# The first chain reordered on every engine, with unread TensorE products in its waits, GpSimd's share of two base inverses recut, and half blocks transposed in turns

## The reference

```python
def _attn_ref(q, k, v, beta):                 # 4 batches, 8 heads, 768 tokens, head dim 48
    k_n = k / (np.linalg.norm(k, axis=-1, keepdims=True) + 1e-06)
    state = np.zeros((B, H, D, D)); y = np.zeros_like(q)
    for t in range(S):
        kt, vt, bt = (k_n[:, :, t], v[:, :, t], beta[:, :, t, None])
        y[:, :, t] = np.einsum('bhd,bhde->bhe', q[:, :, t], state)
        v_old = np.einsum('bhde,bhd->bhe', state, kt)
        state = state + bt[:, :, :, None] * np.einsum('bhd,bhe->bhde', kt, vt - v_old)
    return y
def _moe_ref(x, w1, w2, w3, w_out):           # x 3072 x 384, inner 768
    h = np.maximum(np.maximum(x @ w1, x @ w2), x @ w3)
    return h @ w_out
def _moe2_ref(x, w_gate, w_noise, noise, w1, w2):   # 8 experts, inner 1024
    noisy = x @ w_gate + np.log1p(np.exp(x @ w_noise)) * noise
    # the two best experts of each token, softmax weights over the two,
    # out[token] += weight * (relu(x @ w1[e]) @ w2[e])
```

## Time and profile before

| what | value |
|---|---|
| median of 3 runs | 1051.75 us (1051.23 to 1052.74) |
| the profiled execution: its time | 1057.48 us |
| its span, first to last instruction | 1055.7 us |
| mean granted clock of TensorE | 0.971 of full |
| PE busy | 998.3 us (95%), 10317 matmuls |
| DVE busy | 731.3 us (69%) |
| ACT busy | 475.3 us (45%) |
| POOL busy | 202.0 us (19%) |

### The profile page before, as it was taken

One profiled execution on the slowest core, in us unless ns is written; L12 is line 12 of the kernel. 1 busy time (PEld: TensorE's weight loads), 2 busy tenths in 40 slices (PEclk: granted clock), 3 DMA queues, 4 the chain that ended last, 5 costly groups with the idle time before them and its releaser, 6 DMA issues.

```text
span 1055.7 us, 25602 instructions
## 1 busy us (share of the span) xinstructions
PE 998.3 (95%) x10317; PEld 928.0 (88%) x10317; DVE 731.3 (69%) x1690; ACT 475.3 (45%) x707; POOL 202.0 (19%) x226
## 2 busy tenths in 40 slices
PE   5779988999999999999999999999999999999995
PEld 5667777889889889889899999999999999999994
DVE  5956596487578588442559776777677776776774
ACT  3511424423523523422255464556465464655553
POOL 0086000020022021022306312112111112212111
PEclk8589999999999999999999999999999999999998
DMA  9160131151141042025555645225162525536121
GB/s 320 45 161 2 37 87 21 45 142 21 31 140 37 2 113 52 6 75 200 181 195 188 141 95 152 62 44 173 31 172 46 150 53 165 162 56 165 38 38 23
DMA packets 71459, 102.03 MB, mean 97 GB/s; under 512 B 28624, under 2 KB 59856, under 8 KB 70992
## 3 DMA queue, kind: packets, MB, share of 16 engines
q1 hardware_dynamic: 59296, 78.51, 24.7%
q0 software_dynamic: 10992, 20.70, 10.3%
q10 hardware_dynamic: 1088, 1.65, 0.5%
HBM read 140.53 MB, written 29.51 MB: 161 GB/s over the span
## 4 chain that ended last, share of the span: by engine, by line
PE 84%; DVE 5%; ACT 4%; issue 2%; SPq 2%; DMA 2%; POOLq 0%; DVEq 0%; ACTq 0%
PE ps L1615 40%; PE ps L1761 21%; PE ps L1656 7%; PE ps L1498 3%; PE ps L1592 2%; PE ps L1582 2%; PE ps L1572 2%; PE ps L1672 2%; PE ps L1481 2%; PE ps L1533 1%; PE ps L1543 1%; SPq L446 1%; DVE joint L1040 1%; DMA noise_s<-in_noise 1%; PE ps L1602 1%
## 5 line engine op out<-in xcount | busy, mean ns | idle before, releaser
L1615 PE MATMUL ps<-xr,wr_in 128*128 128x512 f32 x972 | 239.0, 400 | 2.2 <-DVE xr L1070 2.1
L1761 PE MATMUL ps<-w2r,hbT 128*128 128x384 f32 x1320 | 237.0, 337 | 0.0
L1761 PEld LDWEIGHTS ps<-w2r,hbT 128*128 128x128 f32 x1320 | 227.9, 188 | 1.4 <-DVE hbT L1290 1.4
L1615 PEld LDWEIGHTS ps<-xr,wr_in 128*128 128x128 f32 x972 | 180.7, 190 | 42.6 <-DVE xr L1070 2.4
L1615 PE MATMUL ps<-xbT,w1r 128*128 128x256 f32 x1728 | 211.0, 283 | 0.0
L1615 PEld LDWEIGHTS ps<-xbT,w1r 128*128 128x128 f32 x1728 | 210.1, 192 | 0.0
L661 POOL DMA_INDIRECT out_rows<-yb,idx x55 | 90.5, 1646 | 379.8 <-DVE yb L1302 290.9
L1116 DVE TENSOR_TENSOR w1r<-w1s,w1r 128x768 fp32r<-128x768 f32 x128 | 121.2, 957 | 20.0 <-ACT w1r L798 17.7
L814 ACT ACTIVATE hbT<-ps 128x512 fp32r<-128x512 f32 x96 | 57.3, 597 | 169.2 <-PE ps L1615 166.8
L798 ACT CAST w1r<-w1s 128x768 fp32r<-128x768 f32 x128 | 104.4, 827 | 25.5 <-DMA w1s<-in_we 25.5
L1116 DVE TENSOR_TENSOR w2r<-w2s,w2r 128x768 fp32r<-128x768 f32 x128 | 113.8, 951 | 1.5 <-ACT w2r L802 1.5
(11 more groups left out here) (211 smaller groups left out, 1053.3 us busy)
## 6 DMA issues: line engine op xcount, KB each, us to landing
w1s<-in_we SPq DMA_DIRECT2D x32, 1536.0 KB
w2s<-in_we SPq DMA_DIRECT2D x32, 1536.0 KB
xb<-rows SPq DMA_DIRECT2D x25, 402.0 KB
kv_s<-in_kv SPq DMA_DIRECT2D x24, 384.0 KB, 3.3
k_s<-in_k SPq DMA_DIRECT2D x12, 512.0 KB, 3.7
joint<-in_q SPq DMA_DIRECT2D x24, 256.0 KB
out_rows<-padrow SPq DMA_DIRECT2D x13, 384.0 KB, 4.3
w_in<-in_w_blocks SPq DMA_DIRECT2D x3, 1152.0 KB, 12.0
```

Of the source, the lines that this page charges most:

```text
L1615: mm = pe.matmul(dst, w, m, start=(n == 0), stop=(n == len(todo) - 1))
L1761: mm = pe.matmul(ps[:, 6 + h, 0:MD], hbT[:, a, f, h * P:h * P + P], w2r[par][:, b, f], start=(f == 0 and n == 0), stop=(f == FT2 - 1 and n ...
```

## The change

In the opening the lists of all engines are put in another order, and TensorE gets `keep_warm` products: matmuls of a matrix of ones with itself into PSUM banks that nobody reads then. VectorE takes one half of the corner's copy (`corner_half`), ScalarE both halves of the copies after `solve_u(0)` and `outputs(0)`. `fold` no longer waits for the noise, and its loads are issued ahead of the first weights. GpSimd does the first 16 steps of pair 1's base and the first 24 of pair 2's (`POOL_STEPS`), VectorE the rest. In tile 0 the pair's work starts one slot later (`START`), and k1, u1 and s1 stand one slot earlier after it. The first product of tile 0 takes its high parts before the low parts are there. In half blocks `block_rows` stands between the two groups of transposes, and the output product takes the high parts first. The diff, cut to its core:

```diff
+        POOL_STEPS = {1: 16, 2: 24}
+        def base_before(cp):
+            return sum(STEPS - base_ops(POOL_STEPS.get(n, 0)) for n in range(cp))
+        def pool_base_before(cp):
+            return sum(2 * POOL_STEPS.get(n, 0) for n in range(cp))
-        START = {0: 7, 1: 1}
+        START = {0: 8, 1: 1}
-            tight = {... "u0": 6, "s0": 7, "k1": 9, "u1": 10, "s1": 11}
+            tight = {... "u0": 6, "s0": 7, "k1": 8, "u1": 9, "s1": 10}
         def base_done(n, t, i):
-            low, first = place(n - 1, "low"), place(n - 2, "gram1") + (3 if n == 2 else 4)
-            early = Q - 1 if n == 2 else 28
+            low, first = place(n - 1, "low"), place(n - 2, "gram1") + 4
+            early = POOL_STEPS.get(n, 28)
+            if t == 0 and n == 1:
+                return early + (Q - 1 - early) * min(max(i - 1, 0), low - 2) // (low - 2)
# SyncE: w_oT and w_gn now ahead of w_in (w_gn's semaphore is s_wT)
+            sp.dma_start(w_oT[:], w_out_t.rearrange("(k p) f -> p k f", p=P)).then_inc(s_wT, 16)
+            sp.dma_start(w_gn[:], w_gate_noise).then_inc(s_wT, 16)
             for f in range(0, FT, 2):
                 sp.dma_start(w_in[:, f:f + 2], w_blocks[:, f:f + 2]).then_inc(s_w, 16)
-            sp.dma_start(w_oT[:], ...).then_inc(s_wT, 16)
-            sp.dma_start(w_gn[:], w_gate_noise).then_inc(s_noise, 16)
# GpSimd: ones set first; base in parts
+            nc.gpsimd.memset(ones[:], 1.0).then_inc(s_padrow, 1)
-            def second_pair_base():
-                for k in range(Q - 1):
+            def pool_base(cp):
+                for k in range(POOL_STEPS[cp]):
-                if t == -1:
-                    second_pair_base()
+                if t + 2 in POOL_STEPS:
+                    pool_base(t + 2)
# ScalarE
-                for h_ in range(1 if c < 2 else 2):      # u_out, y_out
+                for h_ in range(1 if c == 1 else 2):
             solve_diagonals(0)
+            corner(0)                                    # one half of two
+            off_diagonals_of(3)
             off_diagonals_of(2)
-            off_diagonals_of(3)
             roots(1)
-            corner(0)
# VectorE
+            def corner_half():
+                dve.wait_ge(p_corner, 1)
+                dve.wait_ge(s_solve, 1)
+                rows = slice(L, L + Q)
+                nc.vector.tensor_scalar(by_bank_pair(solve[rows, :, Q:L]), ps[rows, E_BANKS:E_BANKS + 2, :]..., -1.0, None, ALU.mult)
             columns_of(0)
             norm_columns(0)
             scaled_v(0)
+            rows_of(1)
+            corner_half()
             pT_out(0)
-            rows_of(1)
+            norms(1)
             weights_low(0)
-            norms(1)
-            u_half(0)
             state_out(0)
-            y_half(0)
+            weights_low(1)
             scaled_v(1)
             r_out(1)
             pT_out(1)
             u_half(1)
             norm_columns(1)
+            weights_low(2)
             state_out(1)
-            weights_low(1)
             y_half(1)
+            weights_low(3)
             x_low(0)
-                    if t == 0 and n == 0 and f + 2 < FT:
-                        weights_low(f + 2)
+                    if t == 0 and n == 0 and f + 4 < FT:
+                        weights_low(f + 4)
# TensorE
+            def keep_warm(bank, n, step=None):
+                if step is not None:
+                    pe.wait_ge(s_base, base_ops(step))
+                for _ in range(n):
+                    pe.matmul(ps[:, bank, 0:P], ones[:], ones[:], start=True, stop=True)
+                if t == 0 and i == 0:                    # h_product
+                    pe.wait_ge(s_xh, 2)
+                    product(ps[:, 0], pairs, [(0, 0), (1, 0)], closes=False)
+                    pe.wait_ge(s_xr, 2)
+                    product(ps[:, 0], pairs, [(0, 1)], opens=False).then_inc(p_h, 1)
+            pe.wait_ge(s_padrow, 1)
+            keep_warm(D_BANKS, 8)
             gram(0) ... gram(3)
             fold()
+            for k in range(18, Q - 2):
+                keep_warm(E_BANKS + 1, 2, k)
+            keep_warm(E_BANKS + 1, 8, Q - 2)
+            low_times_inverse(0)
+            keep_warm(C_BANKS, 4)
+            corner(0)
             first_k_q()
-            low_times_inverse(0)
-            corner(0)
             solve_u(0)
+            keep_warm(E_BANKS, 6)
             state_step(0)
             outputs(0)
             k_state_and_q(1)
+            keep_warm(H_BANKS, 3)
             solve_u(1)
+            keep_warm(H_BANKS, 3)
             state_step(1)
             outputs(1)
+            keep_warm(H_BANKS, 4)
             to_xT(0, 0)
             to_xT(0, 1)
+            keep_warm(H_BANKS, 4)
# half blocks
+            def half_expert_out(j, par):
+                for g in range(2):
+                    for a, low_parts in ((0, (0, 1)), (1, (0,))):
+                        pe.wait_ge(s_g if a else s_gh, j * 4 + (2 * g + 2))
+                        for f in range(4 * g, 4 * g + 4):
+                            for b in low_parts:
+                                mm = pe.matmul(ps[:, 6, 0:MD], hbT[:, a, f, 0:P], w2r[par][:, b, f], ...)
                     half_h(group, 0)
+                    block_rows(j + 1, 1 - par, next_half)
                     half_h(group, 1)
```

More of the change, by code:

```diff
@@ L401, in place @@
                       "s1": 13}
-            tight = {"low": 1, "corner": 2, "gram0": 3, "gram1": 4, "k0": 5, "u0": 6, "s0": 7, "k1": 9, "u1": 10,
-                     "s1": 11}
+            tight = {"low": 1, "corner": 2, "gram0": 3, "gram1": 4, "k0": 5, "u0": 6, "s0": 7, "k1": 8, "u1": 9,
+                     "s1": 10}
             if name == "xT":
@@ L1042, in pT_out @@
                 last.then_inc(s_pT, 1)
+            def corner_half():
+                dve.wait_ge(p_corner, 1)
+                dve.wait_ge(s_solve, 1)
+                rows = slice(L, L + Q)
+                nc.vector.tensor_scalar(
+                    by_bank_pair(solve[rows, :, Q:L]),
+                    ps[rows, E_BANKS:E_BANKS + 2, :].rearrange("p g (a t) -> p g a t", t=Q), -1.0, None, ALU.mult
+                    ).then_inc(s_corner, 1)
             def u_half(c):
@@ L1526, in low_times_inverse @@
                 elif cp == 1:
-                    pe.wait_ge(s_corner, 1)
+                    pe.wait_ge(s_corner, 2)
                 else:
@@ L1608, in _, with product @@
             PASSES = [(0, 0), (0, 1), (1, 0)]
-            def product(dst, pairs):
-                todo = [(w(a), m(b)) for w, m in pairs for a, b in PASSES]
+            def product(dst, pairs, passes=None, opens=True, closes=True):
+                todo = [(w(a), m(b)) for w, m in pairs for a, b in passes or PASSES]
                 for n, (w, m) in enumerate(todo):
-                    mm = pe.matmul(dst, w, m, start=(n == 0), stop=(n == len(todo) - 1))
+                    mm = pe.matmul(dst, w, m, start=(opens and n == 0), stop=(closes and n == len(todo) - 1))
                 return mm
@@ L1629, in h_product @@
                 f, n = divmod(i, 3)
-                if i == 0:
+                if i == 0 and t:
                     pe.wait_ge(s_xr, 2 * t + 2)
@@ L1747, in half_h, with expert_out @@
                 mm.then_inc(p_g, 2)
-            def expert_out(j, par, half):
-                for h in range(1 if half else 2):
+            def expert_out(j, par):
+                for h in range(2):
                     if isinstance(j, int) and j == 0 and h == 1:
@@ L1755, in expert_out @@
                     for f in range(FT2):
-                        if half and f % 4 == 0:
-                            pe.wait_ge(s_g, j * 4 + (f // 2 + 2))
-                        elif not half and h == 0 and f % 2 == 0:
+                        if h == 0 and f % 2 == 0:
                             pe.wait_ge(s_g, j * 4 + (f // 2 + 1))
@@ L1780, in routed @@
                     pe.wait_ge(s_x2, SUB * T)
-                block_rows(j + 1, 1 - par, next_half)
+                if not half:
+                    block_rows(j + 1, 1 - par, next_half)
                 pe.wait_ge(s_w2r, j * 4 + 4)
@@ L1787, in routed @@
                     pe.wait_ge(s_yb, j * 2)
-                expert_out(j, par, half)
+                if half:
+                    half_expert_out(j, par)
+                else:
+                    expert_out(j, par)
             blocks(pe, routed)
```

70 lines of the change are left out of this document (37 added, 33 removed).

## The result

The changed kernel took 1044.95 us (median of 4 runs, 1044.59 to 1046.82), the kernel before 1051.49 (4 runs, 1051.10 to 1052.74): a ratio of 0.9939, interval 0.9922 to 0.9957. The forecast was 1044.4.

A forecast was written before the change was run, and what follows sets the result against it. TensorE holds 84% of the chain, and in the opening it waits for a chain through all engines. 6.2 us left at pair 2's low product plus 1.1 from half blocks gave 7.3: median 1051.75 to 1044.4, range 1039 to 1050.

The forecast's parts named there:

- Opening: Up to tile 0's start: warm products and new order start tile 0 at 73.3, 7.7 us earlier; bounds 5 and 9.5.
- Tile 0 and pair 1: Tile 0 to tile 1: VectorE full, pair 1's low product plus 3.3 us, then about 3.9 us won up to tile 1.
- rival C: Tile 0: VectorE is not the bound, pair 1's low product follows product 9 at once; 1039 us; with all below 1042, 0.15.
- A: Opening and tile 0: the clock stays low until it would have risen anyway; costs 7.7 us, 1052.1, no change; whole, 0.07.
- 1.3 longer: Between pair 1's low product and tile 1: the state step waits 1.3 us longer.
- Pair 2: Tile 1: GpSimd's 24 steps end 90.4 after tile 0's start, needed at 90.1; loss 0, bounds 0 and 3 us.
- Rival B: Pair 2's base: GpSimd is late; steps taking 1.4 times the row's lose 13.8 us, 1058.2; B and worse, 0.06.
- From there on as before: From pair 2's low product on: order unchanged, 6.2 us remaining there, nothing more won or lost until the half blocks.
- Half blocks: Experts' half blocks: PE's wait for the relu goes with `block_rows` in between; 1.1 us won, bounds 0 and 2.
- minus 0.4: Last half block: second transposes end 0.4 us later and VectorE's list behind them sets the end, losing 0.4.

The follow-up runs named there:

- `pool_old`: Changed kernel with all 31 base steps of pair 1 on GpSimd, pair 2's on VectorE, and tile 0's old slots: 1055.83 us, ratio 0.9991 to the kernel before.
- the timed pair: Changed kernel with its half blocks put back as before, against the changed kernel itself: 1050.50 us, 1.4 above.
- the two repeats: The changed kernel timed again, unaltered, against the kernel before in two later groups: 1049.07 us (ratio 0.9934) and 1050.07 us (0.9939).

## Why the prediction was right, step by step

**Opening: confirmed.** Grams -1.8 by their end against the -1.3 taken; the low product at 39.45 (39.95); the corner's end 45.3 (45.45); `k_state_and_q(1)` at 57.1 (57.6). Tile 0 at 72.66 and 71.84 in the two clean profiles, 74.54 in the one with the fall, against 73.3. Two terms inside were off and cancelled: `weights_low(0)` took 1.6 and not 2.2, with GpSimd's small first steps beside it slowed instead (0.39 to 0.48 us each, where those of pair 2 took 0.24 to 0.29), and `weights_low(2)` and (3) took 2.5 and 2.7. `weights_low(1)` took 1.48; beside it GpSimd's instruction was the one that was held up (3.42 us for a subtract, at 55.85). That is no longer on the path to `k_state_and_q(1)`. The Trainium skill, SBUF — State Buffer, section Who interferes with whom, has the loser of the shared port wait out the other's instruction. The run agrees at 55.85; at 66.43 it doesn't show as turns of that kind, since there both engines are slowed: VectorE takes 2.49 over three instructions that took 1.48 where GpSimd was the one held up, and GpSimd's three steps beside it 0.80 to 0.83 each, about 0.2 us longer than the same steps of pair 2. One engine waiting out the other in full would make some 3.3 us of these six.

**Tile 0 and pair 1: confirmed.** VectorE is full and sets the start of the low product: 24.4 after tile 0's start (24.3 forecast), with PE waiting 2.33 (some 3 forecast). That falls rival C. A's largest term, tile 0's clock, was sized too high: 81 matmuls at full clock take 18.7 us (75 in 17.29 in `pool_old`) and not 18.3, so it was 1.6 and not 2.0; with VectorE setting the low product it should count for nothing here, which no run tests. From there to tile 1, 63.0 (63.3 forecast), with the two stalls gone; the two other profiles took 64.5 and 64.4, for 1.5 us more at half clock in each. The wait of the state step at 130.42 is 2.12 us, 0.75 before: the "1.3 longer" of the forecast.

**Pair 2: confirmed.** GpSimd's 24 steps took 31.8 us (33.8 forecast) and ended 90.1 after tile 0's start, where 90.4 was forecast and 90.1 given as the point from which each microsecond late is lost. The chain of waits runs through all 24 steps, and VectorE is idle for 3.64 us in front of its own. But hardly anything was lost by it: behind those first steps VectorE's list has the maximum of tile 1's second product, which came 4.43 us after the tile's start. In the changed kernel's second profile GpSimd was 1.8 us earlier, counted from tile 1's start; VectorE then waited for that product instead, and the maximum came at 4.35 and the low product at 8.90 (8.98 in the first):

```profile
165.75 0.69 DVE L1104 TENSOR_TENSOR h<-ps,h 128x512 f32<-128x512 f32 x1 [1.61 <-PE ps L1641]
```

(VectorE's timeline of that profile.) So fewer steps on GpSimd would win about 0.1 us at this place, an estimate from these two profiles, and GpSimd's part ended just at the point from which a delay costs. From tile 1's start to the low product 8.98 (9.1). At pair 2's low product 5.2 us were left (6.2 forecast), 5.9 and 6.6 in the two profiles without the fall at 57. Rival B did not come.

**From there on as before: not quite.** In the first profiles the corner of pair 2 starts 6.7 us after the low product in both kernels, set by ScalarE's copy, and something runs at half clock behind it in both: before, PE waited 2.26 us there and lost 1.5 behind it; after, the half-clock product in front filled most of that wait, and the one behind the corner lost 1.6. In the second and third profiles of the changed kernel nothing behind the corner is slow, and the gram stands 11.8 and 11.3 us behind the low product, where before it was 12.7: 0.9 and 1.3 us that the sum had at nil.

**Half blocks: right in mechanism, sized low.** No wait for the relu is left; the profiles show 1.7 to 2.0 us and the timed pair 1.4, against 1.1. The step is "minus 0.4" for the tail with 0.2 a block: the blocks gave 0.33 each and the first 0.63, less 0.33 at the end.

**The whole.** Against the first span of before the change is worth 7.1 (without the 5.1 above), 9.2 and 10.4 us in its three profiles, and by the medians 6.5 us in the first measurement and 7.3 and 6.9 in the two repeats; the forecast of 7.3 lies at the upper end of the medians and the lower end of the profiles. Its weak step was one that it did not have: the price of a wait was taken as its length. Behind the waits of 2.3 us in front of the 32 x 32 products came 1.5 to 3.2 us more at half clock, part of it under waits that were there anyway, and behind the one of 5.8 came 3.8 more. No fall stood in the sum for tiles 0 and 1; the forecast held in spite of it, since without a fall in it the opening brought 8.3 and 9.2 us and not 7.7, and the half blocks 1.7 to 2.0 and not 1.1. That these cancel to within a microsecond is luck; the path, the waits and the order of the engines are not.

## What to carry to other kernels

When two engines end a stretch together, a gain ahead of it is worth only what the slower of them follows: price the edit that speeds up one list and the edit that shortens the other as one, as all the rest of this change without the recut gave 0.6 us, and with it 7.3 (two kernels beside each other). Where PE waits for a full engine, look for work in that engine's list that nothing in the stretch reads; moving one such piece out gave 3 us by the medians and 1.8 by the profiles, where the piece itself takes 1.5. Unread products pay under waits that PE has anyway and in front of narrow work (4.65 us here); under the waits in front of the two low products they kept the clock up in one place and not in the other, and the kernel was no faster. Read the clock behind every wait: here one of 2 us could cost as much again at half clock.

## What was not expected of the hardware

- The granted clock reads 1.00 in the first microseconds of a record, though the work goes at half pace: 27 of TensorE's instructions, most of them of the opening's grams, ran in the window 4 to 6 us and 74 in 6 to 8, both at 1.00; before the change it was 44 in each of 6 to 8 and 8 to 10, at 1.00 too, and the two grams took 6.70 us against 4.16 later; and the first eight unread products (16 records) took 3.78 us where eight records of the later ones took 1.16. The first windows (kernel after):

```profile
4.00:6.00 2.00, 2.00 (x27) 1.77 (x27) 0.31 (x3) 0.00 (x0) 0.00 (x0) 1.00 1.02 384
6.00:8.00 2.00, 2.00 (x74) 2.00 (x74) 0.00 (x0) 0.55 (x1) 0.00 (x0) 1.00 1.00 401
```

- After PE's 5.80 us wait the clock stayed at 0.50 through low product, product and corner, some 10 us, with PE busy for all of it.
- VectorE and GpSimd slow each other by amounts that change with what runs: the same three VectorE instructions took 1.48 to 2.87 us beside GpSimd (2.87 at 83.66 in `pool_old`), and the same subtract of GpSimd's over 87 columns 0.35 us alone and 3.42 beside them.
